# Two attention units moved by half a step, 1e-9 added through a reduce, and four unread products before one transpose

## The reference, cut to what matters

```
scores = q @ k.T / sqrt(64)              # per head, 8 heads of 64
scores = where(mask, scores, -1e9)       # half the heads: the last 32 positions; half: equal position mod 32
attn   = exp(scores - max(scores))
attn   = attn / (sum(attn) + 1e-9)       # the 1e-9 that the change adds in another way
x      = attn @ v
h      = x @ w_in                        # 512 -> 2048
g      = where(h >= 1, h, where(h <= -1, 0, (h + 1)**2 / 4))
y      = g @ w_out                       # 2048 -> 512
out    = y + gate * expert(y)  where y @ w_skip > 0, else y
```

## Time and profile before

| | us |
|---|---|
| median of 3 runs | 508.34 |
| lowest, highest | 508.17, 508.83 |
| the profiled execution's own time | 509.94 |
| its span, first to last instruction | 508.1 |
| TensorE (PE) busy | 497.4 |
| VectorE (DVE) busy | 260.7 |
| GpSimd (POOL) busy | 213.2 |
| ScalarE (ACT) busy | 195.5 |
| mean granted TensorE clock | 0.993 |

### The profile page before, as it was taken

One profiled execution on the slowest core, in us unless ns is written; L12 is line 12 of the kernel. 1 busy time (PEld: TensorE's weight loads), 2 busy tenths in 40 slices (PEclk: granted clock), 3 DMA queues, 4 the chain that ended last, 5 costly groups with the idle time before them and its releaser, 6 DMA issues.

```text
span 508.1 us, 8892 instructions
## 1 busy us (share of the span) xinstructions
PE 497.4 (98%) x3423; PEld 428.7 (84%) x3423; DVE 260.7 (51%) x594; ACT 195.5 (38%) x435; POOL 213.2 (42%) x235
## 2 busy tenths in 40 slices
PE   8899999899999999999999999999999999999996
PEld 5577888789998888888888888888998899888895
DVE  5967557744335525676643676762435242332322
ACT  4776564462223334434332434433322222322222
POOL 0669777662223235455523546551222322222221
PEclk9799999999999999999999999999999999999999
DMA  8993202101101204020310420000210008750001
GB/s 254 337 386 136 76 2 79 53 2 72 54 0 50 73 23 168 13 73 32 97 48 0 173 80 18 17 1 19 88 37 1 1 9 323 275 182 1 2 1 65
DMA packets 18977, 42.15 MB, mean 83 GB/s; under 512 B 2054, under 2 KB 3920, under 8 KB 18932
## 3 DMA queue, kind: packets, MB, share of 16 engines
q1 hardware_dynamic: 18836, 41.54, 23.8%
q0 software_dynamic: 96, 0.02, 0.0%
HBM read 32.94 MB, written 8.78 MB: 82 GB/s over the span
## 4 chain that ended last, share of the span: by engine, by line
PE 85%; DVE 9%; issue 2%; ACT 2%; POOL 0%; DVEq 0%; ACTq 0%
PE bank L1029 36%; PE bank L1045 36%; PE bank L868 4%; PE bank L831 3%; PE bank L848 3%; DVE row_sum L1190 1%; PE bank L812 1%; DVE row_max L1168 1%; DVE x_lo L1200 1%; ACT x_hi L1575 1%; DVE row_sum L1193 1%; PE bank L972 1%; PE bank L953 1%; DVE act_f L1411 1%; DVE bank L1173 1%
## 5 line engine op out<-in xcount | busy, mean ns | idle before, releaser
L1780 POOL TENSOR_TENSOR g_lo<-act_f,g_hi 128x384 fp32r<-128x384 f32 x96 | 97.4, 1014 | 196.9 <-ACT g_hi L1677 196.5
L1668 ACT ACTIVATE act_f<-act_f,half_col 128x384 f32<-128x384 f32 x96 | 59.3, 617 | 201.5 <-DVE act_f L1411 201.5
L1411 DVE TENSOR_SCALAR act_f<-bank 128x384 f32<-128x384 f32 x96 | 53.2, 554 | 143.2 <-PE bank L1029 135.0
L1029 PE MATMUL bank<-x_hi,win_hi 128*128 128x384 f32 x384 | 87.8, 348 | 0.6 <-DVE act_f L1414 0.6
L1045 PE MATMUL bank<-wout_hi,g_hi 128*128 128x512 f32 x285 | 85.1, 407 | 0.0
L1677 ACT CAST g_hi<-act_f 128x384 fp32r<-128x384 f32 x96 | 49.4, 514 | 91.5 <-DVE act_f L1414 91.3
L1029 PE MATMUL bank<-x_hi,win_lo 128*128 128x384 f32 x384 | 83.9, 337 | 0.0
L1029 PE MATMUL bank<-x_lo,win_hi 128*128 128x384 f32 x384 | 83.1, 334 | 0.0
L1045 PE MATMUL bank<-wout_lo,g_hi 128*128 128x512 f32 x285 | 81.0, 392 | 0.0
L1045 PE MATMUL bank<-wout_hi,g_lo 128*128 128x512 f32 x285 | 81.0, 392 | 0.0
L1029 PEld LDWEIGHTS bank<-x_hi,win_hi 128*128 128x128 f32 x384 | 66.6, 188 | 8.5 <-issue 1.5
(11 more groups left out here) (129 smaller groups left out, 431.1 us busy)
## 6 DMA issues: line engine op xcount, KB each, us to landing
w_early<-in_w_dram SPq DMA_DIRECT2D x4, 2048.0 KB, 8.8
qk<-in_qk_dram SPq DMA_DIRECT2D x12, 592.0 KB, 4.6
out_dram<-y_rows SPq DMA_DIRECT2D x18, 256.0 KB, 2.6
win_raw<-in_w_in_dram SPq DMA_DIRECT2D x16, 256.0 KB, 9.3
wout_raw<-in_w_out_dram SPq DMA_DIRECT2D x16, 256.0 KB, 9.8
y_dram<-y_rows SPq DMA_DIRECT2D x15, 256.0 KB, 3.0
v<-in_v_dram SPq DMA_DIRECT2D x6, 384.0 KB
v<-in_v_dram SPq DMA_DIRECT2D x6, 288.0 KB
```

Source lines behind the costliest of these rows:

```text
L1029: mm = pe.matmul(h_ps[s % 2][:, 0:CH], w[:, f, P * k:P * (k + 1)], x[:, k, cols], start=(at == 0), stop=(at == len(order) - 1))
L1411: dve.tensor_scalar(tile, h_ps[s % 2][:, 0:CH], -1.0, 1.0, ALU.max, ALU.min).then_inc(clip_ready, 1)
L1668: act.activation(tile, tile, ACT.Square, bias=half_col[:, 0:1], scale=0.5).then_inc(square_ready, 1)
L1780: pool.tensor_tensor(g_lo[:, s % RING, :], act_f[:, s % 2, :], g_hi[:, s % RING, :].bitcast(F32), ALU.subtract).then_inc(g_lo_ready, 1)
```

## The change

- In `FILLERS` the entry ("P", 1): 4 is new: four unread products are issued ahead of P1, after its first bank has been taken and before the wait for its probabilities.
- Unit 8 goes from half step 6 to 7, with all its jobs one later: S 7, X 8, E 9, P 12, V 14.
- Unit 12 goes from half step 21 to 20 with S 20, X 21, E 22, while P stays at 26 and V at 28.
- The two row sums of a unit are written into every second element of a new buffer `sum_terms`, whose other elements hold 1e-9; a reduce over the pairs then writes `row_sum`. One instruction replaces one instruction. The buffer is filled once at the start by VectorE, which waits for it there.

```diff
-FILLERS = {("P", 0): 4, ("S", 1): 4, ("S", 2): 9, ("P", 2): 5, ...}
+FILLERS = {("P", 0): 4, ("S", 1): 4, ("S", 2): 9, ("P", 1): 4, ("P", 2): 5, ...}
...
-        for i, at in enumerate((6, 10, 14, 17, 21, 24)):
-            unit_at(N_PRO + REST + i, at, 5, 7)
+        for i, at in enumerate((7, 10, 14, 17, 20, 24)):
+            unit_at(N_PRO + REST + i, at, 6 if i == 4 else 5, 8 if i == 4 else 7)
...
+        sum_terms = sb("sum_terms", [TQ, 2, 4, 2], F32)
...
-                    dve.tensor_reduce(sums_of(u, hh), tiled(u, hh), AX.X, ALU.add).then_inc(sum_steps, 1)
+                    dve.tensor_reduce(sum_terms[0:unit_rows(u), hh, 0:u.nt, 0], tiled(u, hh), AX.X, ALU.add)\
+                       .then_inc(sum_steps, 1)
...
-                dve.tensor_scalar(sums, sums, 1e-9, None, ALU.add).then_inc(sum_steps, 1)
+                dve.tensor_reduce(sums, sum_terms[0:unit_rows(u), :, 0:u.nt, :], AX.X, ALU.add).then_inc(sum_steps, 1)
...
+            dve.memset(sum_terms[:, :, :, :], 1e-9).then_inc(terms_ready, 1)
+            dve.wait_ge(terms_ready, 1)
             dve.wait_ge(mask_l_loaded, 16)
```

More of the change, by code:

```diff
@@ L113 @@
 POOL_BEFORE = "G0 G1 G2 G3 G4 G5 R0 R1 R2"
-FILLERS = {("P", 0): 4, ("S", 1): 4, ("S", 2): 9, ("P", 2): 5, ("P", 3): 2, ("P", 4): 2, ("P", 5): 2, ("V", 4): 2}
+FILLERS = {("P", 0): 4, ("S", 1): 4, ("S", 2): 9, ("P", 1): 4, ("P", 2): 5, ("P", 3): 2, ("P", 4): 2, ("P", 5): 2, ("V", 4): 2}
 def jobs_of(names):
@@ L437, in build @@
         mask_l_loaded, mask_s_loaded = sem("mask_l_loaded"), sem("mask_s_loaded")
-        half_ready = sem("half_ready")
+        half_ready, terms_ready = sem("half_ready"), sem("terms_ready")
         warm_ready = sem("warm_ready")
```

## The result

| | median us | lowest to highest | runs |
|---|---|---|---|
| the kernel before | 508.56 | 507.92 to 509.96 | 20 |
| the changed kernel | 509.90 | 509.40 to 510.17 | 20 |

The ratio is 1.0022, with a 95% interval of 1.0016 to 1.0028: the change makes the kernel slower by 1.3 us, where 506.8 was forecast. Its profiled execution took 509.91 us, at a span of 508.1.

What follows compares the result with a forecast made beforehand. TensorE, busy 98%, bounds the kernel; only its idle or low-clock time in the first 105 us can be won. Waits removed 2.5, new 2.4, clock 1.4: 1.5 us less, 508.34 to 506.8, range 504.9 to 508.7.

Steps and rivals of the forecast that it cites:

- The step that failed: VectorE's start: filling the new buffer and waiting for it falls where VectorE waits anyway, so it was counted as free.
- four rivals: Clock falls, 508.2 (0.25); new waits absent, 504.4 (0.15); clock fall put off, 508.1 (0.09); products at half clock, 509.2 (0.08).
- Clock: Prologue, 17 to 24 us: four unread products keep TensorE at full clock, hidden(0) and end 1.4 us earlier.
- Unit 8: First chunk: one half step later removes a 0.95 us TensorE wait and adds waits of 0.4 and 1.3 us.
- Unit 12: First chunk: one half step earlier removes a 1.52 us TensorE wait and adds one of 0.7 us.
- Reduce: VectorE's 1e-9 by a reduce of 0.17 us: worth about 0.5 us alone, about 0 beside the move.
- E3: Prologue, unit 3's slow add of 1e-9, excess 0.5 us: claimed early enough ahead of VectorE's later work.
- The sum: Whole kernel: removed waits 2.5, new waits 2.4, clock 1.4, together 1.5 us less, 508.34 to 506.8.
- 0.04 at P12: First chunk, transposes of unit 12: what the reduce still gains beside the move, 0.04 us.
- Rival (c): Prologue: the clock fall is only put off, low until about 27 us; hidden(0) gains 0.1, total 508.1; chance 0.09.

## Why the prediction was wrong

**The step that failed.** "The buffer's memset and its wait stand ahead of M0 while VectorE waits for S0; nothing else is queued there but M0, and that is 4 us away." As time beside the work this is right, and the memset cost nothing there. But the sum had no term for what an added instruction does to the end of the program. It is 3.07 us between VectorE's branch and its drain (3.67 less 0.60) and 2.6 at the end of the span (5.29 behind `left_i` less 2.65), since SyncE drains 0.5 us after VectorE in the kernel before. All four rivals lacked it too. The forecast stopped at the last products, and the views that it went by have no row behind `left_i`; but that the span goes on for 2.6 us there was to be seen.

**Clock: mechanism right, its worth mis-sized.** This is the second step that failed. The clock held, by the windows and rows above, and hidden(0) came 1.78 us earlier (forecast 1.4). Counted from the first instruction for the 1e-9, the one of unit 0 (at 12.32 in the kernel before, 12.51 with the products alone and 12.35 in the changed kernel), it is 1.60 for the products and 0.21 more by the rest of the change. But I took the profiled execution's 1.6 us above the median as a constant difference between profile and run. It was this very stretch of low clock: the profiled execution had it, most of the runs behind the median had not. Against the median of before the products are worth 0.2 us (508.56 to 508.35), and nothing against its lower cluster in the same group (508.37), where 1.4 was forecast. The sum should have been made from the cluster of the median; the median and the mean clock of 0.993 stood side by side in the table.

**Unit 8: right, and a net loss.** 0.95 removed, 0.43 and 1.20 new (forecast 0.4 and 1.3): together 0.7 lost; 0.85 by the runs, 0.58 by the stretch from hidden(0) to hidden(14). The forecast had this number and let it vanish in the sum of both moves. The larger new wait, P9's, was not a price of moving unit 8 but of moving its value products from 13 to 14.

**Unit 12: right.** 1.52 removed, 0.53 new (0.7). With the reduce there it is worth 0.33 by the runs and 0.40 by the stretch, since the reduce alone takes 0.55 of the 1.52.

**Reduce: duration right, its worth taken for nothing.** Duration 166 ns against 170 forecast. Its worth was 0.45 us and not 0, and two readings of the prediction failed. E3 was not "early enough": its add of 0.68 us stood on the chain to hidden(0). Counted again from the instruction of unit 0, hidden(0) comes 16.90 or 16.91 us later in the three kernels that have the old add and whose clock held (products alone, two memsets more, no reduce), and 16.67 to 16.73 in the seven with the reduce: 0.2 us. And behind hidden(14), where I had held that nothing can be won, the kernel without the reduce takes 0.2 more (401.47 to 401.24). All of it arises between hidden(56) and hidden(57). There an add of 0.85 us and the reciprocal stand ahead of the clip L1411, in VectorE's timeline of the kernel before:

```profile
314.43 0.86 DVE L1193 TENSOR_SCALAR row_sum<-row_sum 96x6 f32<-96x6 f32 x1
...
315.75 0.56 DVE L1411 TENSOR_SCALAR act_f<-bank 128x384 f32<-128x384 f32 x1 [0.25 <-issue]
```

The 0.2 is not the add's alone, though. The kernels with one memset more, two more and one fewer have the same long add there, but not the 0.25 us of idle time behind it, and lose nothing; the three with 829 records and the old add have both. What the 0.25 is stays open.

**The sum.** Waits removed 0.95 + 1.52 = 2.47, new 0.43 + 1.20 + 0.53 = 2.16: 0.3 won, with about the same in the kernel without the reduce (0.44 + 1.21 + 0.57). The stretch from hidden(0) to hidden(14) is shorter by 0.57 to 0.64. Most of the rest is at P12, as the busy time of one row and not as idle time. Before and after, in TensorE's timeline:

```profile
101.09 0.92 PE L848 MATMUL bank<-ident,prob 96*128 96x96 f32 x6
```
```profile
98.93 0.66 PE L849 MATMUL bank<-ident,prob 96*128 96x96 f32 x6
```

Before, P12's fourth transpose starts 0.28 us behind the third, where the others are 0.08 to 0.14 apart, because M13's last L1180 had started only 0.09 us ahead of it. By the two rows that is about 0.25 us, where the prediction had "0.04 at P12". In all the work of the profiled execution is 2.68 shorter, where 1.5 was forecast, and the end of the program takes all of it back. With the end short the changed kernel takes 507.32, 0.5 above the forecast; with it long, 509.90. That 507.32 would lie in the stated range is luck in part: 1.4 was counted for a clock that most runs had already, and 0.1 for the moves and the reduce, which are worth about 1.1 against the lower cluster (508.4 to 507.3).

**Rival (c)** drew on what the Trainium skill, "TensorE: Matmul & The Clock Gate", Part 4, PE-mode transpose, says, that transposes don't count as busy for the clock as products do. The clock held through P1, V0 and P2 in the profiles of all nine kernels with the four products. That doesn't test the rule, since it also held in most runs of the kernel before.

## What to carry to other kernels

Look at the end of a program before and after a change: the time from the last computed value to the span's end should be the same in both, and if it isn't, count each engine's instructions. In this program, which ends by a jump over code that isn't run, one instruction more on one engine cost some 3 us there; moving one setup instruction to an engine that had room took it back, at no price that was seen. And before a profile's excess over the median is carried along as a constant, see whether the stretch that the change works on is what makes the difference. A wait within a group of the timeline shows as a longer row and not in brackets, so compare a group's busy time too.

## What was unexpected of the hardware

- From a branch over skipped code to the drain behind it VectorE took 0.60 to 0.61 us in ten traces and 3.67 to 3.93 in three; one instruction more on VectorE decided between them.
- The same program is granted different clocks in the prologue. Of 20 runs of the kernel before 16 lay at 507.9 to 508.9 and 4 at 509.8 to 510.0; with four unread products all twelve runs of the products-only kernel fell within 507.94 to 508.69. In one experiment a wait of 1.86 us of TensorE at 89.2 to 91.05 was followed by 3.4 us at a granted clock of 0.52, where the waits of 1.50 to 1.52 of the other kernels at the same place had no fall behind them in their profiles.
- At the same clip of VectorE, near 315 us, three kernels with 829 records show 0.25 us of idle time behind a long add and its reciprocal; the kernels with 828, 830 and 831 records and the same add show none.
- An add in place of 8 elements a partition took up to 1239 ns beside a GpSimd instruction, a reduce of 16 elements at the same place never more than 167 ns.
